# A fused attention and two expert layers on one core: scores four groups ahead, four probability buffers, another order of loads, and the first matrix products among the last groups

## The reference

```python
def _attn_ref(q, k, v):                       # 2 batches, 8 heads, 768 tokens, 64 features
    k_sum = k.reshape(B, H, nb, 32, D).max(axis=3)
    v_sum = v.reshape(B, H, nb, 32, D).mean(axis=3)
    scores_l = scale * q @ k.T                # kept where |i - j| < 16, else -1e9
    scores_s = scale * q @ k_sum.T + log(32)
    a = softmax(concatenate([scores_l, scores_s], axis=-1))
    return a @ concatenate([v, v_sum])
def _moe_ref(x, w_in, w_out):                 # 1536 tokens, 512 features, 2048 hidden
    h = np.maximum(x @ w_in, 0.0)
    return h * h @ w_out
def _moe2_ref(x, w_in, w_out, a, b):
    h = x @ w_in
    P = a[0] + a[1]*h + a[2]*h**2 + a[3]*h**3
    Q = 1.0 + |b[0]| * |h| + |b[1]| * h**2
    return (P / (Q + 1e-06)) @ w_out
```

## Time and profile before

| | |
|---|---|
| median of 3 runs | 616.96 us (616.08 to 617.96) |
| the profiled execution | 617.14 us, span 615.4 us |
| busy share of the span | PE 95%, DVE 72%, ACT 42%, POOL 24% |
| 24 groups of attention | from the first scores at 5.8 us to the last output at about 84 us |
| chain that ended last | PE 47%, DVE 36%, issue 9%, ACT 3%, DMA 2% |
| sizes of one DMA | vwin 576 KB, kraw 400 KB, q 384 KB, weight slot 512 KB, spread 36 KB |

### The profile page before, as it was taken

How to read it: one execution, slowest core, us unless ns; L and a number is a source line. 1 busy time by engine, 2 the same in 40 slices (tenths; PEclk the granted TensorE clock), 3 DMA queues, 4 the chain that set the end, 5 groups by cost and what they waited for, 6 DMA issues and landing times.

```text
span 615.4 us, 9725 instructions
## 1 busy us (share of the span) xinstructions
PE 582.0 (95%) x3360; PEld 472.8 (77%) x3360; DVE 444.0 (72%) x834; ACT 261.3 (42%) x553; POOL 145.1 (24%) x150
## 2 busy tenths in 40 slices
PE   4788699999999999999999989999999999999995
PEld 3556578888888888888888867788888888888884
DVE  4678787665343233456675699999999999999996
ACT  3778611111031111311111855556766566766564
POOL 5556610000030000210000656522221222221220
PEclk9999999999999999999999999999999999999999
DMA  8788433000000000022333200000100000100001
GB/s 232 212 261 251 129 128 148 0 1 0 1 0 0 0 0 0 0 81 91 103 102 103 69 1 0 1 0 1 68 0 0 0 0 0 68 1 0 1 2 68
DMA packets 12351, 32.68 MB, mean 53 GB/s; under 512 B 1568, under 2 KB 3872, under 8 KB 12320
## 3 DMA queue, kind: packets, MB, share of 16 engines
q1 hardware_dynamic: 12320, 32.25, 16.8%
HBM read 27.92 MB, written 3.15 MB: 50 GB/s over the span
## 4 chain that ended last, share of the span: by engine, by line
PE 47%; DVE 36%; issue 9%; ACT 3%; DMA 2%; DVEq 1%; POOL 1%; SPq 1%; POOLq 0%
PE bank L499 22%; PE bank L544 21%; DVE ratio L927 9%; DVE numer L909 6%; DVE ratio L921 5%; DVE numer L907 5%; DVE ratio L916 5%; DVE hhi L934 4%; ACT prob L617 2%; DMA vwin<-vsum 2%; PE bank L468 1%; PE bank L449 1%; PE bank L485 1%; PE bank L459 1%; SPq L250 1%
## 5 line engine op out<-in xcount | busy, mean ns | idle before, releaser
L499 PE MATMUL bank<-xhi,whi 128*128 (+1 forms) x384 | 150.3, 391 | 0.3 <-DVE wlo L820 0.3
L499 PE MATMUL bank<-xlo,whi 128*128 (+1 forms) x384 | 149.9, 390 | 0.0
L499 PE MATMUL bank<-xhi,wlo 128*128 (+1 forms) x384 | 149.8, 390 | 0.0
L630 ACT ACTIVATE hsq<-bank 128x512 f32<-128x512 f32 x48 | 28.8, 600 | 218.5 <-PE bank L499 218.5
L409 POOL TENSOR_TENSOR denom<-denom,habs 128x512 f32<-128x512 f32 (+1 forms) x49 | 62.3, 1272 | 250.9 <-ACT denom L686 250.9
L499 PEld LDWEIGHTS bank<-xhi,whi 128*128 128x128 f32 x384 | 72.5, 189 | 15.9 <-DVE wlo L820 0.7
L499 PEld LDWEIGHTS bank<-xhi,wlo 128*128 128x128 f32 x384 | 72.3, 188 | 15.1
L499 PEld LDWEIGHTS bank<-xlo,whi 128*128 128x128 f32 x384 | 72.4, 189 | 14.9
L559 PE MATMUL bank<-whi,hhi 128*128 128x512 f32 x192 | 75.9, 395 | 7.6 <-DVE hlo L938 7.6
L559 PE MATMUL bank<-whi,hlo 128*128 128x512 f32 x192 | 74.8, 390 | 0.0
L559 PE MATMUL bank<-wlo,hhi 128*128 128x512 f32 x192 | 74.8, 389 | 0.0
(11 more groups left out here) (65 smaller groups left out, 858.9 us busy)
## 6 DMA issues: line engine op xcount, KB each, us to landing
wraw<-w SPq DMA_DIRECT2D x32, 512.0 KB, 4.1
vwin<-vw SPq DMA_DIRECT2D x8, 576.0 KB, 5.4
kraw<-kT SPq DMA_DIRECT2D x8, 400.0 KB, 6.0
q<-qT SPq DMA_DIRECT2D x8, 384.0 KB, 6.4
out<-osb SPq DMA_DIRECT2D x12, 256.0 KB, 2.1
vwin<-vsum SPq DMA_DIRECT2D x32, 36.0 KB
ca<-coef_a SPq DMA_DIRECT2D x1, 2.0 KB, 10.7
braw<-coef_b SPq DMA_DIRECT2D x1, 1.0 KB, 11.8
```

The costliest lines, as they stand in the source:

```text
L499: last = mm(hps[j % 2][:, :], W[a][:, j, kt * P:(kt + 1) * P], X[b][:, kt, bass.ds(CH * c, CH)], start=k == 0, stop=k == 3 * KT - 1)
```

## The change

Four probability buffers instead of three, and four buffers of vwin. PE makes scores(G + 4), ACT exps(G + 3), DVE guard and invert of G + 2 in one piece and masked(G + 4), POOL normalise(G + 2), each in its iteration G. Summaries are made in groups 1, 3, 5, 8, 11, 14 and 17 and not in groups 0, 3, 6, ... 18; each is copied in the same group.

SP issues the loads in another order: the first k in thirds (one of them on ACT's queue), vwin(0) ahead of k(1), vwin(2) and k(3) ahead of the first spreads, vwin three heads ahead, and the spreads of head n + 2 at the end of iteration n. Keys are no longer padded in memory; DVE clears the edges of kraw. ACT makes the means matrix. The coefficients are loaded later.

The hidden tiles 0 and 1 are made in quarters in PE's iterations 20 to 23. POOL splits w_in of slots 0 to 2 in pieces of 256 columns in its iterations 17 to 22, and DVE splits w_out of these slots in its iterations 21 to 23.

```diff
-P_RING = 3
+P_RING = 4
 RING = 3
+V_RING = 4
+THIRD = S // GPB
+SPLIT_FROM = GROUPS - 7
+SUMMARY_AT = [0, 1, 3] + [GPB * n - 4 for n in range(3, NB)]
...
-            sp.dma_start(kraw[n % RING][:, :], kT[n]).then_inc(k_in[n % RING], 16)
+            sp.dma_start(kraw[n % RING][:, BAND:BAND + S], kT[n]).then_inc(k_in[n % RING], 16)
+        def load_k_first(i):
+            sp.dma_start(kraw[0][:, BAND + THIRD * i:BAND + THIRD * (i + 1)],
+                         kT[0][:, THIRD * i:THIRD * (i + 1)]).then_inc(k_first[i], 16)
...
-            if n >= RING:
-                sp.wait_ge(o_done, done(2, GPB * (n - RING + 1) - 1))
+            if n >= V_RING:
+                sp.wait_ge(o_done, done(2, GPB * (n - V_RING + 1) - 1))
...
-        load_k(0)
+        load_k_first(0)
+        load_k_first(2)
         load_q(0)
+        load_vwin(0)
         load_k(1)
-        load_vwin(0)
         load_q(1)
+        load_k(2)
         load_vwin(1)
-        load_k(2)
         load_q(2)
-        sp.dma_start(ca[:, :], coef_a.partition_broadcast(P)).then_inc(coef_in, 16)
-        sp.dma_start(braw[:, :], coef_b.partition_broadcast(P)).then_inc(coef_in, 16)
-        spread_summary(0)
         for n in range(NB):
-            if n + 2 < NB:
-                load_vwin(n + 2)
+            if n == 0:
+                load_vwin(2)
+            elif n + RING < NB:
+                load_vwin(n + RING)
             if n + RING < NB:
                 load_k(n + RING)
+            if n == 0:
+                spread_summary(0)
+                load_vwin(RING)
+                spread_summary(1)
+            if n + RING < NB:
                 load_q(n + RING)
             if 2 <= n < 2 + EARLY:
                 load_first(n - 2)
...
-            if n + 1 < NB:
-                spread_summary(n + 1)
+            if n == 1:
+                spread_summary(2)
+            if 0 < n and n + 2 < NB:
+                spread_summary(n + 2)
```

POOL and PE:

```diff
+        normalise(1, 1)
+        def split_in(x):
+            j, part = x // 2, SLOT // 4 * (x % 2)
+            index = slice(None), j, slice(part, part + SLOT // 4)
+            split(index, w_hi_pool, x, w_in_ready)
         for G in range(GROUPS):
             n, gi = divmod(G, GPB)
-            if G + 1 < GROUPS:
-                normalise(G + 1, (G + 1) % P_RING)
-            if n + 2 < NB:
+            if G + 2 < GROUPS:
+                normalise(G + 2, (G + 2) % P_RING)
+            if G == 1:
+                load_windows(2)
+                spread_all(2)
+            if 1 <= n < NB - 2:
                 if gi == 0:
                     load_windows(n + 2)
                 elif gi == 1:
                     spread_all(n + 2)
+            x = G - SPLIT_FROM
+            if x == 0:
+                pool.wait_ge(w_first, 16 * EARLY)
+            if 0 <= x < 2 * EARLY:
+                split_in(x)
...
+        def hidden_first(j, kt):
+            pe.wait_ge(w_in_ready, 2 * j + kt // 2 + 1)
+            if kt == 0:
+                pe.wait_ge(s_free, done(2, GROUPS - 1))
+            pe.wait_ge(xlo_done, done(2, XPAIRS - NCH if kt == KT - 1 else NCH * kt))
+            hidden(0, j, j, (kt,))
+        early = {GROUPS - 4: [(0, 0), (0, 1)], GROUPS - 3: [(0, 2), (1, 0)],
+                 GROUPS - 2: [(0, 3), (1, 1)], GROUPS - 1: [(1, 2), (1, 3)]}
         scores(0)
         scores(1)
+        scores(2)
         pe.wait_ge(means_done, 1)
         summary(0)
-        scores(2)
         for G in range(GROUPS):
             turn(G, G % P_RING)
-            if G + P_RING < GROUPS:
-                scores(G + P_RING)
-            if G % GPB == 0 and G // GPB + 1 < NB:
-                summary(G // GPB + 1)
...
+            for ahead in (3, 4) if G == 0 else (4,):
+                if G + ahead < GROUPS:
+                    scores(G + ahead)
+            for n in range(1, NB):
+                if SUMMARY_AT[n] == G:
+                    summary(n)
+            for j, kt in early.get(G, ()):
+                hidden_first(j, kt)
             output(G)
```

ACT and DVE:

```diff
+        act.dma_start(kraw[0][:, BAND + THIRD:BAND + 2 * THIRD], kT[0][:, THIRD:2 * THIRD]).then_inc(k_first[1], 16)
+        for j in range(GPB):
+            last = a.copy(means[:, j, 2 * j:2 * j + 2], mean[:, :])
...
         exps(0, 0)
+        exps(1, 1)
         copy_summary(0)
-        exps(1, 1)
+        exps(2, 2)
...
-            if G + 2 < GROUPS:
-                exps(G + 2, (G + 2) % P_RING)
+            if G + 3 < GROUPS:
+                exps(G + 3, (G + 3) % P_RING)
...
+        for r in range(RING):
+            d.memset(kraw[r][:, 0:BAND], 0.0)
+            last = d.memset(kraw[r][:, BAND + S:], 0.0)
+        last.then_inc(edges, 1)
...
         make_mask()
-        block_max(0, 0, GPB)
-        make_means()
+        for part in range(GPB):
+            block_max(0, part, 1)
         masked(0)
-        block_max(1, 0, GPB)
         masked(1)
         guard(0)
         invert(0)
         masked(2)
+        block_max(1, 0, GPB)
+        guard(1)
+        invert(1)
         for G in range(GROUPS):
-            if G + 1 < GROUPS:
-                guard(G + 1)
+            if G + 2 < GROUPS:
+                guard(G + 2)
+                invert(G + 2)
             if G >= 2:
                 (x_lo if G % 2 else x_hi)(G // 2 - 1)
-            if G + 1 < GROUPS:
-                invert(G + 1)
...
+            if G == 1:
+                block_max(2, 0, GPB)
+            for n in range(3, NB):
+                part = G - GPB * (n - 2) + 1
+                if 0 <= part < GPB:
+                    block_max(n, part, 1)
+            for ahead in (3, 4) if G == 0 else (4,):
+                if G + ahead < GROUPS:
+                    masked(G + ahead)
+            if G >= GROUPS - EARLY:
+                split_out(G - GROUPS + EARLY)
```

More of the change, by code:

```diff
@@ L54 @@
 EARLY = PAIRS - 1
-DVE_FIRST = 2
 LATE = 4
@@ L130, in build @@
     ksum = [places[1](f"ksum{r}", [P, NBLK]) for r in range(RING)]
+    prob = [places[1](f"prob{i}", [P, GU, COLS]) for i in range(P_RING)]
     assert all(a.offset <= w + 2 * half for a, w in zip(places, (W_HI, W_LO)))
     area = Area(WORK)
-    prob = [area(f"prob{i}", [P, GU, COLS]) for i in range(P_RING)]
     probT = [area(f"probT{i}", [COLS, GU * P]) for i in range(2)]
+    vwin.append(area("vwin3", [COLS, NW, P]))
     mask = area("mask", [P, 3, COLS])
@@ L165, in build @@
     q_in = [sem(f"q_in{r}") for r in range(RING)]
+    k_first = [sem(f"k_first{i}") for i in range(GPB)]
     k_in = [sem(f"k_in{r}") for r in range(RING)]
-    vw_in = [sem(f"vw_in{r}") for r in range(RING)]
-    vsum_in = [sem(f"vsum_in{r}") for r in range(RING)]
+    vw_in = [sem(f"vw_in{r}") for r in range(V_RING)]
+    vsum_in = [sem(f"vsum_in{r}") for r in range(V_RING)]
     coef_in = sem("coef_in")
@@ L249, in spread_summary @@
                 rows = KW + 2 * GPB * t
-                sp.dma_start(vwin[n % RING][rows:rows + 2 * GPB, :, :],
+                sp.dma_start(vwin[n % V_RING][rows:rows + 2 * GPB, :, :],
                              vsum[n % 2][32 * t:32 * t + 2 * GPB, :].unsqueeze(1).to_broadcast([2 * GPB, NW, P])
-                             ).then_inc(vsum_in[n % RING], 16)
+                             ).then_inc(vsum_in[n % V_RING], 16)
         def load_first(j):
@@ L458, in summary @@
                 for t in range(4):
-                    last = mm(vps[32 * t:32 * t + 32, 0:P], means[:, j, :], vwin[n % RING][0:KW, GPB * t + j, :],
+                    last = mm(vps[32 * t:32 * t + 32, 0:P], means[:, j, :], vwin[n % V_RING][0:KW, GPB * t + j, :],
                               start=j == 0, stop=j == GPB - 1)
@@ L491, in _, with hidden @@
         W, X, HID = (whi, wlo), (xhi, xlo), (hhi, hlo)
[L493 to L498, removed]
+        def hidden(c, j, n, kts=range(KT)):
+            if kts[0] == 0:
+                pe.wait_ge(h_free, done(2, n - 2))
+            for kt in kts:
+                for i, (a, b) in enumerate(PARTS):
                     last = mm(hps[j % 2][:, :], W[a][:, j, kt * P:(kt + 1) * P],
-                              X[b][:, kt, bass.ds(CH * c, CH)], start=k == 0, stop=k == 3 * KT - 1)
-                    k += 1
-            last.then_inc(h_full, 1)
+                              X[b][:, kt, bass.ds(CH * c, CH)], start=kt == 0 and i == 0, stop=kt == KT - 1 and i == 2)
+            if kts[-1] == KT - 1:
+                last.then_inc(h_full, 1)
         def weights_ready(index):
[L505 to L508, removed]
+            if index < EARLY:
+                pe.wait_ge(w_in_ready, 2 * (index + 1))
             elif index >= 2 * FT - LATE:
@@ L537, in sum_b @@
             pe.wait_ge(g_ready, done(2, n))
+            if j < EARLY:
+                pe.wait_ge(w_out_ready, j + 1)
             for dt in range(KT):
@@ L638, in _ @@
             a.copy(probT[G % 2][:, :], tps[0:COLS, :]).then_inc(probT_done, 1)
-            if G + 2 < GROUPS:
-                exps(G + 2, (G + 2) % P_RING)
+            if G + 3 < GROUPS:
```

(19 more changed lines are left out.)

84 lines of the change are left out of this document (38 added, 46 removed).

## The result

The changed kernel took 622.66 us as the median of eight runs, the kernel before 617.73 us beside it: a ratio of 1.0077 (95% interval 1.0048 to 1.0105). I had forecast 613.6 us in 606 to 618.

A forecast was written before the change was run, and what follows sets the result against it. Latencies, chiefly a 4.80 us turn covering two groups, were taken to bound the attention, PE's work the rest. End +7.5, start -5.1, middle +0.9 made 3.3 us, so 613.6 us, in a range of 606 to 618.

The forecast's parts named there:

- the waits that I named as signs: Attention: PE waiting for spreads at a first output near 21 us and near 30; ksum for kraw 2 to 4 us.
- a gain of 7.5: End of the attention, from out(17): 15.4 us instead of 22.9, with hidden products in quarters in groups 20 to 23.
- a loss of 5.1: Start of the attention: out(5) at 35.3 us instead of 30.2, bounds 3.7 and 7.0.
- the half clock's 1.2 us: Start, behind out(0): after PE idles some 6 us, a half clock would add 1.2 us at most.
- I take 21.3: Start: out(0) at 21.3 us instead of 18.46, as the first spreads queue behind 0.93 MB more loads; bounds 20.2 and 22.6.
- I take 9.6, so out(3): Start: out(3) follows out(0) by 9.6 us through the chain of summary(1), so at 30.9 us against 25.81.
- Its maxima are asked for by DVE in group 3m-7 ... Landed k to that group's copy ... six groups: Middle: the turn through the load of k takes 9.4 us plus landing, 15.2 us for six groups, 2.5 each.
- My landing of 5.8: Middle: a load of k lands 5.8 us after issue, bounds 5.1 and 7.0.
- a gain of 0.9: Middle: groups 5 to 17 take 30.4 us instead of 31.3, bounds +2.3 and -1.5.
- An iteration there has no scores ... 2.65 us: End: each iteration of groups 20 to 23, with two quarters of a large product, takes 2.65 us.
- Rival A: Whole attention: spreads overtake loads, out(0) stays at 18.5, DMA limits at 2.2 us a group, time 607.0; chance 0.20.
- Rival C: Middle: SP's queue never empty, k lands after 9 us, six groups take 18.4 us, time 620.0; chance 0.12.

The follow-up runs named there:

- e10: The changed kernel with vwin(3) issued behind the spreads of head 1 instead of between those of heads 0 and 1; ratio 1.0098 to the kernel before.
- e1: The changed kernel with the four spreads of head 0 issued ahead of vwin(2) and k(3) instead of behind them; ratio 0.9980 to the kernel before.
- e3: The changed kernel with k issued one iteration earlier from head 5 on, ahead of the spreads; ratio 1.0065 to the kernel before.
- e4: The changed kernel with the edits of e1, e2 and e3 together; ratio 0.9937 to the kernel before.
- e2: As e1, with summary(1) also made and copied in group 0, ahead of out(0), its spreads behind q(3); ratio 0.9938 to the kernel before.
- e5: The kernel before with the lead alone: four probability buffers, scores four ahead, exponentials three, normalisation two; ratio 0.9978 to the kernel before.

## Why the prediction was wrong

Most of the mechanisms were there: of the waits that I named as signs, out(0) waited 8.14 us, the one near 30 came at 34.28 with 0.45, and ksum waited for kraw by 1.9, 3.4 and 1.1 us in heads 5 to 7. The sign of the sum was wrong, since a gain of 7.5 stood against a loss of 5.1, and three steps failed to the same side. The start left out vwin(3), shaved the price of the loads and took less than half of the half clock's 1.2 us (3.5 us in all), the middle had the turn over six groups instead of five (2.7 us, not all of it by this turn), and the end had no term for a stop of PE (3.6 us); together 9.8, from 81.1 to 90.9. By its own steps:

- **"I take 21.3" for out(0)**: 23.96, beyond my upper bound of 22.6. I priced 0.93 MB at 246 GB/s. The queue ran at 210 GB/s from 18 to 22 us, and from 0 to 24 us it moved some 5.3 MB: the 4.5 that I counted, the spreads' 0.15, and vwin(3)'s 0.59, issued at 14.9 us behind the spreads. The price of the loads ahead was good before I shaved it: the first packet of the spreads was moved at 18.8 us, 4.0 later than before (14.8), where I had 3.8. I had left vwin(3) out, and it held the spreads for some 2 us more (e10). e1 shows that 5.7 us of out(0) were the order of these DMAs.
- **"I take 9.6, so out(3)"**: 10.3. The chain was right but for the last 0.37 us ahead of the copy of the sums, in which ACT waited for PE's summary(1). The half clock that I had only as a bound came in full: SP issued the spreads 5.0 us after out(0) (28.93 - 23.96) instead of 3.6; the issues took 3.05 and the landing 2.3, near the 3.07 and 2.5 that I had.
- **"Its maxima are asked for by DVE in group 3m-7 ... Landed k to that group's copy ... six groups"**: this step failed. I followed DVE, POOL and PE to the copy of group 3m-4. ACT comes first: exponentials of group 3m-3 stand in its list ahead of the copy of group 3m-5, and they wait for the masks behind the late k. So the turn covers five groups, not six. The chain of waits for head 6:

```profile
45.32 0.57 ACT probT L686
...
47.58 0.77 SPq L261
...
50.69 0.47 SPq L254
...
51.20 6.70 DMA kraw<-kT
...
57.92 0.06 DVE ksum L817
...
59.49 1.32 ACT prob L664 x7
60.81 0.47 ACT probT L686
...
61.33 0.69 PE bank L518 x16
```

The copy of group 8 ends at 45.9, k is issued 5.3 us later, as I had it, lands after 6.7, and 3.4 us behind that out(13) starts: 15.4 us for five groups, 3.1 each. The other two heads fit as well: k(5), issued at 43.41, landed 4.9 us later, and 48.3 + 3.4 is out(10) at 51.73; k(7), issued at 59.98, landed 5.2 us later, and 65.2 + 3.4 is out(16) at 68.63. From the copy that releases the spreads their turns took 13.6 and 15.0 us (in that of k(7) the issue came 6.3 us after the copy, as summary(5) was late and ran at half speed). My landing of 5.8 was good (4.9, 6.7 and 5.2). The three turns overlap, so the stretch lost 1.8 us against before, where I had a gain of 0.9. Part of that is not this turn: behind out(10) PE stood for another 0.64 us until POOL had spread the maxima of head 5 (L350, to 53.54), ran its next groups of matmuls at half speed, and out(11) came 4.2 us later. That the late k is what costs is shown for the waits (7.4 to 2.1 us in e3) and in e4's middle against e2's, not in a ratio.
- **"An iteration there has no scores ... 2.65 us"**: right, 2.59. The end still took 19.0 us instead of 15.4, by the stop of 2.31 us and some 1.3 us of half clock after it. That is what failed in the term: it had PE's work and the weight splits, and put stops of PE at nothing without a word. Nothing in my working looked at what PE itself waits for when no semaphore holds it, though the trace before has such waits ("issue").
- **Rival A**, that the spreads overtake, was wrong: out(0) waited until the loads ahead of it were through. The page of the Trainium skill that I named with it, DMA: Bandwidth & Descriptors, section "Queues, rings and completion order", says only that completion need not be in order. This trace shows no overtaking of the loads by the spreads (the last packet of k(3) ended at 21.3, the last of the spreads at 23.1). It shows the reverse: most packets of vwin(3), issued behind the spreads, were moved ahead of their last one. **Rival C** had the right sign, for the reason that I gave to the forecast: k landed after 4.9 to 6.7 us, not after 9, and the queue was not full (a DMA share of 0.71 from 40 to 60 us).

The half clock behind idle PE, for which I named the Trainium skill's TensorE: Matmul & The Clock Gate, section "Part 1: The HAM clock gate", is borne out in the durations, 1.13 us for out(0) after 8.14 us idle and 1.12 for out(19) after 2.31, and in the granted 0.50 from 78.5 us.

## What to carry to other kernels

More buffers and a longer lead moved nothing that could be told from 1 here by themselves (e5), as the loads go through one queue whose head waits for something late. Place each load by the first instruction that wants it, ask what every waiting DMA holds up behind it, and keep large loads from standing right behind a small one that is wanted at once. When a wait is added, follow it through each engine's own list, not only along the data: here ACT's next copy stood behind exponentials of a group two further on. And where several terms of either sign are summed from one trace, let the range take them all on their bad side.

## What was not expected of the hardware

- PE stopped in scores(23), behind the 13th of its 16 matmuls, for 2.0 to 2.8 us, in five traces (after the change, e1, e3, e4, e10), with no semaphore to wait for.
